# Attention stage with one pair of score banks, four transpose banks and the output matmuls dealt over three tiles

## The reference

```
scores = q @ k.T / sqrt(64) + bias[head]            # bias from a small MLP of |i - j| and i
attn   = exp(scores - rowmax) / (rowsum + 1e-9)
x      = attn @ v, heads side by side               # 2304 x 512
x      = max(x @ w1, x @ w2, x @ w3) @ w_out        # inner size 768
h      = x @ w_in                                   # inner size 2048
out    = where(h >= 1, h, where(h <= -1, 0, (h + 1)^2 / 4)) @ w_out2
```

## Time and profile before

| | us |
|---|---|
| median of 3 runs | 1109.19 |
| lowest and highest | 1108.04 and 1111.84 |
| the profiled execution | 1108.04 |
| its span | 1106.3 |
| TensorE busy in the span | 1048.8 (95%) |
| VectorE, ScalarE, POOL busy | 557.0, 510.1, 313.1 |

### The profile page before, as it was taken

How to read it: one execution, slowest core, us unless ns; L and a number is a source line. 1 busy time by engine, 2 the same in 40 slices (tenths; PEclk the granted TensorE clock), 3 DMA queues, 4 the chain that set the end, 5 groups by cost and what they waited for, 6 DMA issues and landing times.

```text
span 1106.3 us, 18896 instructions
## 1 busy us (share of the span) xinstructions
PE 1048.8 (95%) x6648; PEld 921.8 (83%) x6648; DVE 557.0 (50%) x1313; ACT 510.1 (46%) x1082; POOL 313.1 (28%) x544
## 2 busy tenths in 40 slices
PE   5869999999999889999999999999999999999997
PEld 2348777777777679999999999999998999989996
DVE  8948667766667522322223222675444454444543
ACT  7958666666667443221212122554344343443432
POOL 5028667766767456000000023560000000000000
PEclk9989999999999999999999999999999999999999
DMA  3561241332421134000000011221001010010101
GB/s 129 206 210 44 51 143 34 87 108 51 122 59 42 50 95 133 1 1 0 0 0 0 0 39 57 88 84 29 1 1 28 0 29 0 0 28 0 29 1 29
DMA packets 80798, 55.61 MB, mean 50 GB/s; under 512 B 44896, under 2 KB 66400, under 8 KB 80736
## 3 DMA queue, kind: packets, MB, share of 16 engines
q1 hardware_dynamic: 80736, 54.82, 17.1%
HBM read 39.46 MB, written 15.34 MB: 50 GB/s over the span
## 4 chain that ended last, share of the span: by engine, by line
PE 78%; DVE 8%; issue 6%; DMA 2%; SPq 2%; ACT 2%; POOL 1%; DVEq 1%; ACTq 0%
PE ps L1000 38%; PE ps L1044 18%; PE ps L1012 7%; PE ps L926 4%; PE ps L956 4%; PE ps L944 4%; DVE s_sb L752 3%; DVE xT L715 2%; DMA bias_h<-bias_scratch 2%; DVE k_lo L770 2%; PE ps L911 1%; DVE pt_t L761 1%; ACT probs L577 1%; DVEq L715 1%; SPq L288 1%
## 5 line engine op out<-in xcount | busy, mean ns | idle before, releaser
L1000 PE MATMUL ps<-x_hi,w_hi 128*128 128x384 f32 x816 | 274.6, 336 | 3.8 <-DVE x_lo L792 3.5
L1000 PE MATMUL ps<-x_hi,w_lo 128*128 128x384 f32 x816 | 274.4, 336 | 0.0
L1000 PE MATMUL ps<-x_lo,w_hi 128*128 128x384 f32 x816 | 273.8, 336 | 0.0
L752 DVE CUSTOM_DVE_ANT_0 s_sb<-ps,bias_h 128x576 f32<-128x576 f32 (+1 forms) x160 | 120.1, 752 | 84.5 <-issue 60.5
L502 POOL TENSOR_TENSOR w_lo<-raw,w_hi 128x256 fp32r<-128x256 f32 x108 | 83.5, 805 | 277.4 <-ACT w_hi L611 277.4
L1000 PEld LDWEIGHTS ps<-x_hi,w_hi 128*128 128x128 f32 x816 | 153.8, 188 | 9.1 <-issue 4.0
L1000 PEld LDWEIGHTS ps<-x_lo,w_hi 128*128 128x128 f32 x816 | 153.7, 188 | 3.9
L1000 PEld LDWEIGHTS ps<-x_hi,w_lo 128*128 128x128 f32 x816 | 153.6, 188 | 0.0
L577 ACT ACTIVATE probs<-s_sb,row_min 128x576 f32<-128x576 f32 (+1 forms) x160 | 124.7, 779 | 40.9 <-DVE row_min L752 40.8
L461 POOL TENSOR_SCALAR probs<-probs,row_inv 128x512 f32<-128x512 f32 (+1 forms) x160 | 108.7, 693 | 90.4 <-DVE row_inv L732 88.7
L1044 PE MATMUL ps<-w_hi,g_lo 128*128 128x512 f32 x288 | 113.9, 395 | 0.0
(11 more groups left out here) (95 smaller groups left out, 1662.6 us busy)
## 6 DMA issues: line engine op xcount, KB each, us to landing
bias_scratch<-probs SPq DMA_DIRECT2D x36, 288.0 KB, 2.1
bias_h<-bias_scratch SPq DMA_DIRECT2D x7, 1152.0 KB, 6.6
raw<-in_moe_w_out SPq DMA_DIRECT2D x22, 256.0 KB, 3.1
raw<-in_moe_w SPq DMA_DIRECT2D x18, 256.0 KB, 3.0
out<-o_sb SPq DMA_DIRECT2D x36, 128.0 KB, 2.4
q_in<-in_q SPq DMA_DIRECT2D x32, 128.0 KB, 2.3
k_in<-in_k SPq DMA_DIRECT2D x32, 128.0 KB, 2.4
v_in<-in_v SPq DMA_DIRECT2D x32, 128.0 KB, 2.3
```

Of the source, the lines that this page charges most:

```text
L752: dve.tensor_tensor_reduce(halves(s_sb[0:n, (par + t) % 2, :]), score_ps(m, t)[0:n], halves(bias_h[0:n, par, t, :]), 1.0, 3.0e38, ALU.add, ...
L1000: last = pe.matmul(ps[:, bank, 0:BLK], w[:, at:at + P], x[:, kt, :], start=(kt == 0 and n == 0), stop=(kt == KT - 1 and n == 2))
```

## The change

Scores now use banks 0-1 only, and the scores of a tile wait for the bias addition of the tile just before. The transposed groups take banks 2 to 5 in turn, so a group waits for the one four places earlier in the list. The two output halves have a bank each, 6 and 7, and a half waits for the copy of the same half two steps earlier. Each half is cut into three shares by `kt`: block 0 at t=2, blocks 1 and 2 at t=3, blocks 3 and 4 at t=4. The `qk` transposes work on 64 rows in place of 128 and write 64 columns each.

```diff
-        OUT_AT = NT - 1
-        O_BANK_A = 4
-        O_COLS = (slice(0, O_SPLIT), slice(O_SPLIT, S))
+        SHARES = {2: (0,), 3: (1, 2), 4: (3, 4)}
+        O_BANKS = ((6, slice(0, O_SPLIT)), (7, slice(O_SPLIT, S)))
...
-        T_BANKS = 3
+        T_BANKS = 4
...
-            return 5 + SLOT[m, name] % T_BANKS
+            return 2 + SLOT[m, name] % T_BANKS
...
-        def score_ps(m, t):
-            at = 2 * ((NT * m + t) % 2)
-            return ps[:, at:at + 2, 0:HC]
+        def score_ps():
+            return ps[:, 0:2, 0:HC]
...
-                        if NT * m + t >= 2:
-                            pe.wait_ge(s_bias, NT * m + t - 1)
+                        if m >= 1 or t:
+                            pe.wait_ge(s_bias, NT * m + t)
...
-                                last = pe.transpose(ps[:, bank, n * P:(n + 1) * P],
-                                                    x[:, e, T, :, :].rearrange("p a d -> p (a d)"), ident[:, :])
+                                last = pe.transpose(ps[:, bank, n * HALF:(n + 1) * HALF],
+                                                    x[0:HALF, e, T, :, :].rearrange("p a d -> p (a d)"),
+                                                    ident[0:HALF, 0:HALF])
...
-                    if t == OUT_AT:
-                        if par == 1 and has(m, 3):
-                            outputs((m - 3) // 2, 0)
-                        if par == 0 and has(m, 4):
-                            outputs((m - 4) // 2, 1)
+                    output_share(t)
...
+                def outputs(i, half, kts):
+                    bank, cols = O_BANKS[half]
+                    for kt in kts:
+                        if kt == 0:
+                            if half == 0:
+                                pe.wait_ge(vv_in[i % 2], 64 * (i // 2 + 1))
+                                pe.wait_ge(t_act, ACT_COUNT[2 * i + 2, "p2"])
+                                pe.wait_ge(t_dve, DVE_COUNT[2 * i + 2, "tail"])
+                            if i >= 1:
+                                pe.wait_ge(o_ok, 2 * (i - 1) + half + 1)
```

More of the change, by code:

```diff
@@ L557, in output @@
                 def output(i, half):
-                    cols = O_COLS[half]
+                    bank, cols = O_BANKS[half]
                     act.wait_ge(o_ps, 2 * i + half + 1)
                     act.activation(xT_flat[:, i * S + cols.start:i * S + cols.stop],
-                                   ps[:, O_BANK_A, 0:cols.stop - cols.start], ACT.Copy).then_inc(o_ok, 1)
+                                   ps[:, bank, 0:cols.stop - cols.start], ACT.Copy).then_inc(o_ok, 1)
                 for t in range(NT):
@@ L591, in step @@
                             act.activation(q_s[:, e, MAIN:S], src[:, 0:HALF], ACT.Copy, scale=-SCALE)
-                            act.activation(k_hi[:, e, MAIN:S], src[:, P:P + HALF], ACT.Copy).then_inc(t_act, 1)
+                            act.activation(k_hi[:, e, MAIN:S], src[:, HALF:2 * HALF], ACT.Copy).then_inc(t_act, 1)
                     if t == O_AT:
@@ L600, in _ @@
                 step(m)
+            output_last = PAIRS // 2 - 1
+            bank, cols = O_BANKS[1]
             act.wait_ge(o_ps, PAIRS)
-            act.activation(xT_flat[:, (PAIRS // 2 - 1) * S + O_SPLIT:PAIRS // 2 * S],
-                           ps[:, O_BANK_A, 0:S - O_SPLIT], ACT.Copy).then_inc(o_ok, 1)
+            act.activation(xT_flat[:, output_last * S + cols.start:output_last * S + cols.stop],
+                           ps[:, bank, 0:cols.stop - cols.start], ACT.Copy).then_inc(o_ok, 1)
             act.wait_ge(o_ok, PAIRS)
@@ L752, in step @@
                         dve.tensor_tensor_reduce(
-                            halves(s_sb[0:n, (par + t) % 2, :]), score_ps(m, t)[0:n],
+                            halves(s_sb[0:n, (par + t) % 2, :]), score_ps()[0:n],
                             halves(bias_h[0:n, par, t, :]), 1.0, 3.0e38, ALU.add, ALU.min,
@@ L773, in step @@
                             dve.wait_ge(t_act, ACT_COUNT[m, "qk"])
-                            dve.tensor_tensor(k_lo[:, e, MAIN:S], ps[:, t_bank(m, "qk"), P:P + HALF],
+                            dve.tensor_tensor(k_lo[:, e, MAIN:S], ps[:, t_bank(m, "qk"), HALF:2 * HALF],
                                               k_hi[:, e, MAIN:S].bitcast(F32), ALU.subtract).then_inc(t_dve, 1)
@@ L913, in turn_rows @@
                     last.then_inc(t_ps, 1)
[L915 to L924, removed]
+                def outputs(i, half, kts):
+                    bank, cols = O_BANKS[half]
+                    for kt in kts:
[6 more added lines that the diff above has]
+                                pe.wait_ge(o_ok, 2 * (i - 1) + half + 1)
                         for h in range(2):
-                            last = pe.matmul(ps[h * HALF:(h + 1) * HALF, O_BANK_A, 0:cols.stop - cols.start],
+                            last = pe.matmul(ps[h * HALF:(h + 1) * HALF, bank, 0:cols.stop - cols.start],
                                              v_in[:, i % 2, h, kt, :],
@@ L929, in outputs, with output_share @@
                                              start=(kt == 0), stop=(kt == T))
-                    last.then_inc(o_ps, 1)
+                    if kts[-1] == T:
+                        last.then_inc(o_ps, 1)
+                def output_share(t):
+                    if t not in SHARES:
+                        return
+                    if par == 1 and has(m, 3):
+                        outputs((m - 3) // 2, 0, SHARES[t])
+                    if par == 0 and has(m, 4):
+                        outputs((m - 4) // 2, 1, SHARES[t])
                 if m == -1:
@@ L943, in step @@
                             for c in range(2):
-                                last = pe.matmul(score_ps(m, t)[0:n, c, :], q_s[:, par, t * P:t * P + n],
+                                last = pe.matmul(score_ps()[0:n, c, :], q_s[:, par, t * P:t * P + n],
                                                  kx[:, par, c * HC:(c + 1) * HC],
```

## The result

The changed kernel takes 1125.59 us (median of 4 runs, 1122.12 to 1127.39) against 1108.83 before (median of 4; the table ahead of the prediction has three of these): a ratio of 1.0146, 95% interval 1.0127 to 1.0166. It is slower, as forecast. The profiled execution took 1122.62 us with a span of 1120.8, 14.5 more than before. The sum was made against the profiled execution, and against that 1126.0 is 3.4 too high; that it meets the median within 0.4 is partly luck. The profiled execution is one of the quick ones: of the 24 executions on record, the six with a mean granted clock of 0.991 or more took 1122.1 to 1123.3, and the rest, but for one of 1123.1, took 1125.0 to 1128.3.

What follows compares the result with a forecast made beforehand. TensorE was taken to set the pace, priced by starts of weight loads. 12.7 (14 pairs) + 4.5 (first steps) + 1.0 (reloads) - 0.2 (end) = +18.0 on 1108.04: 1126.0 us, own range 1118 to 1131, overall 1109 to 1134.

Steps and rivals of the forecast that it cites:

- The loop: Scores waiting for the previous tile's bias addition: 1.76 at t=0, 1.68 later, against 1.41 of TensorE work; +0.35 and +0.27 a step.
- The bank waits: Waits of `p3` for `k_lo` and odd-step `p1` for `pt_t` go entirely: 0.72 in even steps, 0.50 + 0.60 in odd.
- The shares: Output half in three groups: the fixed 0.18 of a group paid three times in place of once, +0.36 a step.
- I take no cost for entering: Output shares start behind full-width transposes without delay, argued from 64-row scores loaded before `p3` ended: 0 us.
- the second rival: Entering a share drains too: 0.2 more at t=3 in 28 steps, +5.6, 1131.6 us; chance 0.17.
- qk: At t=2, `qk` transposes on 64 rows cost 0.44 in place of 0.22, with a late load: +0.22 a step.
- The ends: Attention outside steps 3 to 30: steps 0 to 2 about +1.5 each (+4.5), bias reloads +1.0, steps 31, 32 and last half -0.2.
- The reloads of the bias: Around three reloads only one tile of scores can be ready in place of two: about +0.35 each, +1.0.
- The drain: End of attention: step 31 +1.4, step 32 -1.1, last half -0.5, together -0.2.
- That switching is free: Narrow groups overlap what follows and `qk` is not late: 1109.5 us, no change; chance 0.13.
- That the loop is hidden: Bias addition is through within TensorE's own 1.41: -0.51 a pair, -7.1 in all, 1101 us; chance 0.10.
- late VectorE: Loss exceeds the sum through VectorE's late addition 4 or a clock falling in longer waits: about 1140 us; chance 0.08.

Runs made afterwards that it cites:

- One pair alone: Kernel before with scores on banks 0-1 only, each waiting for the bias addition of the tile just before; outputs in one group, three transpose banks: ratio 1.0242.
- the kernel with the early copy: Kernel before with three output shares, one output bank, two score pairs, and ScalarE's copy of the output half at t=0 in place of t=1: ratio 1.0003.
- the reordered kernel: Kernel before with the 64-row scores of t=4 put ahead of `p3` on TensorE, both score pairs kept: ratio 0.9893.
- one reordering: Two runs on the kernel before: VectorE's copy of `tail` ahead of the t=0 bias addition in odd steps, 0.9978; 64-row scores of t=4 ahead of `p3`, 0.9893.
- both: Kernel before with the early VectorE copy of `tail` and the t=4 scores ahead of `p3` together, bias reload not moved: ratio 0.9863.
- the two kernels of the longest steps: Kernel before with one score pair, 1.0242 (steps 10.07 and 11.07); changed kernel with outputs in one group at t=4, 1.025 (steps 10.08 and 11.08).

## Why the prediction was right, point by point

**The bound.** Right: TensorE's program order sets the pace, and pieces priced by the starts of weight loads add up. A pair came out at 20.33 us (predicted 20.32). So close a fit is luck in part: per pair the sum was 0.44 short at t=3 and 0.22 over at t=1 of the odd step, and the rest is in small pieces. The tiles of its odd step add up to 9.74, too, not to the 9.76 written.

**The loop.** Right in place and size: 1.76 at t=0, 1.65 at t=1. The idle time of the held loads is 0.32 and 0.22, below the 0.35 to 0.5 that I had named as its sign. One pair alone costs 2.4%. The 0.2 that I put on t=1 of odd steps was wrong (by its own numbers, 1.70 + 1.04 = 2.74 against 2.61, it should have been 0.13): the copy and the two inverses between the additions take 243.50 to 244.47 = 0.97 from start to start, less than 0.69 + 0.35, because rows of VectorE overlap by some 0.08. The copy also starts with the row of the minimum (243.50), not behind it. They just fit under the scores, which were loaded at 243.64 and, at 0.83 to the addition, would not have let it begin before 244.47.

**The bank waits.** Right that they go. But the experiments say more: with one score pair they would have gone anyway, under the loop. The fourth transpose bank is bought with the second score pair. With the outputs in one group it pays for nothing that the loop does not already hide, and with three shares `p3` does not wait for `k_lo` even with three banks (258.25 in the kernel with the early copy); the fourth bank alone was not tested.

**The shares.** The fixed cost of leaving a narrow group was right. "I take no cost for entering" was the step that failed: the share at t=3 is loaded 0.17 late (248.46 above), so t=3 took 2.18 and 2.40 in place of 1.96 and 2.18. This is what the second rival asserted, at 0.2 a step. The row that I argued from, scores of 64 columns of weights entering free behind `p3`, holds for that pair of operations only. The Trainium skill (TensorEngine Tiling (Array Packing), Key Properties) has the drain at any change of mode. This trace agrees for the outputs on either side of full-width matmuls (0.17 to enter, 0.38 to 0.49 to leave) and for `qk` (0.17). The 64-row scores still entered behind full-width scores without a gap (250.00 in the reordered kernel is 0.51 behind 249.49, the price of any scores), and behind an output share they came 0.39 late (249.48 above), as full-width scores do. By these rows they behave as a full-width piece on both sides, which is why they were the wrong row to price a share with.

**qk.** Mis-sized, +0.22 for a measured +0.04 to +0.05. Its late load of 0.17 is real (246.45), but with `qk` on 128 rows the share behind it is late by the same 0.17 (257.16 in the kernel with the early copy). Here the switch is paid once, by whichever narrow piece comes first. At t=2 the sum was right (2.02 for a measured 2.01) and only its attribution to `qk` wrong. In the odd step the errors of t=3 (+0.22) and t=1 (-0.22) cancel.

**The ends.** The first steps were over-priced, 4.5 for 2.7, and their parts were further off: step 0 took 3.0 more (1.5 predicted), step 1 1.4 less (1.5 more predicted; in the kernel before, its first transposes waited 1.37 for POOL), step 2 1.1 more (8.46, not 8.9). The prediction left out the clock there. Both kernels run a stretch of steps 0 and 1 at half the clock, but the mean granted clock of step 0 is 0.87 before and 0.60 after, of step 1 0.65 and 0.85. So in the changed kernel the loop of step 0 runs at the lower level, where a load takes 0.50 in place of 0.30 and a tile 2.18 in place of 1.65:

```profile
71.00 0.50 PEld L955 LDWEIGHTS ps<-k_hi,q_s 128*128 128x128 f32 x2 [3.62 <-DVE row_min L752]
...
73.18 0.50 PEld L955 LDWEIGHTS ps<-k_hi,q_s 128*128 128x128 f32 x2 [0.41 <-DVE row_min L752]
```

How much of the 2.7 is owed to the clock, no run separates.

The reloads of the bias were signed wrong: longer steps leave the DMA more time, so their excess fell by 0.9 in place of rising by 1.0. The experiments mostly agree, each by its one profiled execution: 5.0 and 4.3 with one reordering and 10 with both (2.7 of it the clock), 1.1 and 1.0 in the two kernels of the longest steps. The kernel with two output groups does not fit, with 4.9; its first reload step took 14.34 at a mean clock of 0.88. The drain was right at -0.2 as a sum: step 31 +1.4 as predicted, step 32 -0.8 for -1.1, the last halves -0.8 for -0.5.

**The rivals.** That switching is free is refuted by the 0.17 and 0.39 in every step, and by t=3 of 2.18 for pieces of 1.82 in the experiment. That the loop is hidden is refuted by the waits at every t=1. No late VectorE appeared, and no falling clock in steps 3 to 30 (granted clock 1.00); in the first two steps it had a part, as said above.

## What to carry to other kernels

Two engines that hand one buffer back and forth run in series; before a second buffer is given away, price the loop (load to consumer's start, consumer, release) against the producer's other work for each tile, 1.65 against 1.41 here, and look for an order of the same instructions that removes the wait in question without it. Put independent work into the gap: one reordering of four matmuls won 1.1%, where the change of banks lost 1.5%. When steps get shorter, look at once at transfers that are issued a fixed number of instructions, not of microseconds, ahead, and at the granted clock behind every longer wait: two of three such waits here cost another 1.3 us each at half the clock.

## What was not expected of the hardware

- TensorE's busy time rose by 27.6 us (1048.8 to 1076.4) with the same matmuls, since held narrow and wide matmuls are shown until a modelled end. Only starts of weight loads showed the loss.
- A switch between full-width and narrow matmuls has a price in both directions here, 0.17 us to enter and 0.38 (256 columns) or 0.49 (320) of load idle to leave, of which about 0.18 is lost, an estimate from the difference of the two widths (the share of one `kt` at t=2 gives 0.58 - 0.425 = 0.16). A 64-column set of score weights behind full-width scores had none.
- Rows of VectorE overlap: the copy of 0.69 us held the engine for 0.61 (243.50 to the next start at 244.11).
